# Attention, routed experts and a PReLU layer on one core: the high and low parts of an expert's tokens in one product, an expert's matrices in two halves of tiles

## The reference

```python
# q, k, v [4, 12, 448, 64]
scores = scale * q @ k.T - log(S)
x = (1 / (1 + exp(-scores))) @ v                    # as [1792, 768]
# eight experts, 224 tokens each, given out by logits x @ w_gate in falling order
h = maximum(x[mask] @ w1[e], 0.0)                   # w1 [8, 768, 1024]
out[mask] = h @ w2[e]                               # w2 [8, 1024, 768]
h = out @ w_in                                      # [768, 2048]
g = maximum(h, 0) + alpha * minimum(h, 0)
return g @ w_out                                    # [2048, 768]
```

## Time and profile before

| | |
|---|---|
| median of 3 runs | 1016.87 us (1015.24 to 1021.43) |
| the profiled execution | 1018.44 us, its span 1016.8 us |
| TensorE busy | 992.3 us of the span, 98% |
| DVE, ACT, POOL busy | 562.4, 397.0, 180.8 us |
| share of the chain that ended last | TensorE 93%, DVE 3%, ACT 2% |
| granted TensorE clock | 0.999 |

### The profile page before, as it was taken

The page is one execution under the profiler, slowest core; times in us unless marked ns, Lnnn a source line. Parts: engine busy times, 40 slices in busy tenths (PEclk is TensorE's granted clock), DMA queues, the critical chain, the costliest instruction groups (busy, mean ns, idle before and its releaser), DMA issues.

```text
span 1016.8 us, 16391 instructions
## 1 busy us (share of the span) xinstructions
PE 992.3 (98%) x6510; PEld 851.8 (84%) x6510; DVE 562.4 (55%) x1282; ACT 397.0 (39%) x642; POOL 180.8 (18%) x197
## 2 busy tenths in 40 slices
PE   7999999898999999999999999999999999999997
PEld 5555555467999999899999999999999999999996
DVE  4444343588678538948852873696358547221212
ACT  5767777511242223455222225531221455222212
POOL 0100000015420101244000024340101425000001
PEclk9999999999999999999999999999999999999999
DMA  9999985347598787676969646579785446976601
GB/s 212 273 277 270 253 259 175 139 154 255 143 322 320 230 190 250 230 185 204 368 235 242 238 146 174 176 267 341 229 241 181 142 129 197 372 244 216 217 1 55
DMA packets 122473, 222.48 MB, mean 219 GB/s; under 512 B 53056, under 2 KB 70752, under 8 KB 122064
## 3 DMA queue, kind: packets, MB, share of 16 engines
q1 hardware_dynamic: 89120, 121.14, 38.0%
q0 software_dynamic: 20304, 90.61, 28.1%
q10 hardware_dynamic: 12976, 9.70, 3.9%
HBM read 184.84 MB, written 36.58 MB: 218 GB/s over the span
## 4 chain that ended last, share of the span: by engine, by line
PE 93%; DVE 3%; ACT 2%; issue 1%; DMA 0%; POOLq 0%; POOL 0%; ACTq 0%; DVEq 0%
PE psum L1012 23%; PE psum L1026 22%; PE psum L959 11%; PE psum L989 10%; PE psum L740 7%; PE psum L724 7%; PE psum L708 2%; PE psum L954 2%; PE psum L984 2%; PE psum L841 1%; DVE hits L1606 1%; PE psum L906 1%; PE psum L766 1%; PE psum L894 1%; PE psum L758 1%
## 5 line engine op out<-in xcount | busy, mean ns | idle before, releaser
L1012 PE MATMUL psum<-y_high,unit 128*128 128x448 f32 x768 | 230.8, 369 | 0.5 <-DVE y_low L1520 0.4
L1026 PE MATMUL psum<-g_high,unit 128*128 128x448 f32 x756 | 228.0, 369 | 0.9 <-DVE g_low L1531 0.9
L1012 PEld LDWEIGHTS psum<-y_high,unit 128*128 128x128 f32 x768 | 144.3, 188 | 13.7 <-issue 1.2
L1026 PEld LDWEIGHTS psum<-g_high,unit 128*128 128x128 f32 x756 | 142.0, 188 | 14.2 <-DVE g_low L1531 1.9
L1012 PE MATMUL psum<-y_low,unit 128*128 128x448 f32 x384 | 140.7, 367 | 0.0
L1026 PE MATMUL psum<-g_low,unit 128*128 128x448 f32 x378 | 138.6, 367 | 0.0
L1210 ACT ACTIVATE above<-psum 128x448 f32<-128x448 f32 x64 | 34.9, 546 | 246.2 <-PE psum L1012 240.5
L1503 DVE TENSOR_TENSOR unit<-raw,unit 128x768 fp32r<-128x768 f32 (+1 forms) x106 | 109.6, 1059 | 38.7 <-ACT unit L1184 30.5
L1526 DVE SCALAR_TENSOR_TENSOR below<-below,neg_alpha,above 128x448 f32<-128x448 f32 x64 | 43.7, 683 | 148.9 <-ACT below L1211 148.7
L959 PE MATMUL psum<-x_high,unit 128*128 128x224 f32 x672 | 117.8, 276 | 1.0 <-issue 1.0
L989 PE MATMUL psum<-h_high,unit 128*128 128x224 f32 x672 | 115.7, 276 | 1.4 <-issue 1.4
(11 more groups left out here) (192 smaller groups left out, 1302.5 us busy)
## 6 DMA issues: line engine op xcount, KB each, us to landing
unit<-ffn_parts SPq DMA_DIRECT2D x120, 768.0 KB, 6.4
ffn_parts<-pre_parts POOLq DMA_DIRECT2D x24, 768.0 KB, 6.8
ffn_parts<-unit SPq DMA_DIRECT2D x8, 768.0 KB, 6.7
q_in<-in_q_dram SPq DMA_DIRECT2D x24, 224.0 KB, 4.7
v_in<-in_v_dram SPq DMA_DIRECT2D x24, 224.0 KB, 6.7
k_in<-in_k_dram SPq DMA_DIRECT2D x23, 224.0 KB, 6.2
pre_raw<-in_moe_w_in_dram ACTq DMA_DIRECT2D x12, 384.0 KB, 6.9
pre_raw<-in_moe_w_out_dram ACTq DMA_DIRECT2D x12, 384.0 KB, 6.3
```

What stands on the lines that cost most here:

```text
L1012: last = pe.matmul(psum[:, in_bank(m), 0:PAIR], w, y[:, c, :], start=(c == 0 and i == 0), stop=(c == DC - 1 and i == 2))
L1026: last = pe.matmul(psum[:, OUT_BANK + d, 0:PAIR], w, g[:, m % 2, :], start=(m == 0 and i == 0), stop=(m == (FC - 1 if q < GROUPS - 1 else ...
```

## The change

- `x_high` and `x_low` become one tile `x_both` with the two parts side by side, `h_high` and `h_low` become `h_both`. For each unit and tile, one product of 448 columns (weights high x both parts) and one of 224 (weights low x tokens high, into the second half of the same bank) take the place of three of 224. A tile of the result fills a bank and stands there as two halves of 224 columns, whose sum is the result.
- A bank now holds one tile, so `hidden` goes in two halves of 4 tiles and `returned` in two halves of 3, each over all units. The second half uses the banks of the first, and its first products wait until DVE has added the two sides of each (`h_added`, `y_added`). Units are given back in the second half only. Units of an expert are needed at twice the rate in a first half.
- DVE adds the two sides: `add_h`, 8 `tensor_reduce` for each expert, `add_y`, 6. Each reads 448 columns of PSUM, hopping between the sides, and writes 224 to SBUF. They stand first in DVE's steps. The relu, the rounding and the rests then read these sums in SBUF. y goes in 6 pieces of 224 columns, not 3 of 448.
- The rank passes have other steps; DVE's and ACT's splits of two steps reach less far ahead; the first row of fillers is 69, not 76; POOL gathers three units of w2 ahead of the second expert's tokens (in the groups after the first).
- Expert 0 and the PReLU layer keep their products.

```diff
-    BUSY_SEARCH, BUSY_FLAGS, BUSY_PLACES, BUSY_VALUES = 76, 11, 14, 10
+    BUSY_SEARCH, BUSY_FLAGS, BUSY_PLACES, BUSY_VALUES = 69, 11, 14, 10
...
-        x_high = [sb(f"x_high{i}", [128, DC, CAP], F32R) for i in range(2)]
-        x_low = [sb(f"x_low{i}", [128, DC, CAP], F32R) for i in range(2)]
+        x_both = [sb(f"x_both{i}", [128, DC, 2, CAP], F32R) for i in range(2)]
-        h_high = sb("h_high", [128, EC, CAP], F32R)
-        h_low = sb("h_low", [128, EC, CAP], F32R)
+        summed_h = ExitStack()
+        h_sums = sb("h_sums", [128, EC, 2, CAP], F32, summed_h)
+        summed_h.close()
+        h_both = sb("h_both", [128, EC, 2, CAP], F32R)
...
+        summed_y = ExitStack()
+        y_sums = sb("y_sums", [128, DC, PAIR], F32, summed_y)
+        summed_y.close()
...
         def prepared(s):
-            return {OWN - 2: OWN + 2, OWN - 1: OWN + 4}.get(s, 0) if s < OWN else s + LEAD + 1
+            if s < OWN:
+                return {OWN - 2: OWN + 2, OWN - 1: OWN + 4}.get(s, 0)
+            return s - s % STEPS + OWN + DC - 2 if s % STEPS in (OWN - 2, OWN - 1) else s + LEAD + 1
         SPLIT = [u for u in range(LAST) if is_own(u) and u >= OWN or is_late(u)]
...
                 if r == 2:
-                    passes, later = (21, 22, 23, 24, 28, 30, 31, 32), (34, 35, 37, 41)
+                    passes, later = (21, 24, 25, 28, 30, 31, 32, 33), (34, 35, 37, 41)
                 elif r == 3:
                     passes, later = (43, 45, 47, 48, 50, 51, 52, 53), (55, 57, 59, STEPS + 5)
                 elif r % 2 == 0:
-                    passes, later = (9, 11, 13, 16, 22, 24, 26, 28), (31, 32, 34, 38)
+                    passes, later = (22, 24, 26, 28, 30, 31, 33, 34), (36, 37, 39, 43)
                 else:
-                    passes, later = range(42, 50), (51, 52, 54, STEPS + 3)
+                    passes, later = (45, 46, 47, 48, 50, 51, 52, 53), (54, 55, 57, STEPS + 4)
                 PASS_AT[r] = [at + i for i in passes]
                 THR_AT[r], FLAGS_AT[r], IDX_AT[r] = [at + i for i in later[0:3]]
...
+            def three_terms(bank, w_high, w_low, both, first, final):
+                def high():
+                    return pe.matmul(psum[:, bank, 0:2 * CAP], w_high, both.rearrange("p a s -> p (a s)"),
+                                     start=first, stop=final, skip_group_check=True)
+                def low():
+                    return pe.matmul(psum[:, bank, CAP:2 * CAP], w_low, both[:, 0, :], start=False, stop=False,
+                                     skip_group_check=True)
+                if final:
+                    low()
+                    return high()
+                high()
+                return low()
+            def hidden(r):
+                M = EC // 2
+                for half in range(2):
+                    for c in range(DC):
+                        u = w1_unit(r, c)
+                        step = step_of(half, c, DC)
+                        if step is not None:
+                            rows_back(w1_unit(r, step))
+                            routing(w1_unit(r, step))
+                        if half == 0:
+                            if c == 0:
+                                if r == 1:
+                                    pe.wait_ge(first_split, DC // 2)
+                                else:
+                                    pe.wait_ge(sel_split, PIECES * (r - 1))
+                                if r % 2 == 0:
+                                    pe.wait_ge(in_taken, FC * (r // 2))
+                                    pe.wait_ge(out_taken, DC * (r // 2 - 1) + M - 1)
+                            pe.wait_ge(w_split, splits(u + 1))
+                        for i in range(M):
+                            m = M * half + i
+                            if half == 1 and c == 0:
+                                pe.wait_ge(h_added, h_sum(r, i))
+                            last = three_terms(H_BANK + i, *part(unit, u, m), x_both[r % 2][:, c], c == 0, c == DC - 1)
+                            if c == DC - 1 and m < EC - 1:
+                                last.then_inc(h_done, 1)
+                        if half == 1:
+                            last.then_inc(unit_used, 1)
+            def returned(r):
+                M = DC // 2
+                for half in range(2):
+                    for c in range(EC):
+                        u = w2_unit(r, c)
+                        step = step_of(half, c, EC)
+                        if step is not None:
+                            routing(w2_unit(r, step))
+                        if half == 0:
+                            if c == 0:
+                                if r == 1:
+                                    pe.wait_ge(y_split, y_ready(0, DC - 1))
+                                elif r % 2 == 1:
+                                    pe.wait_ge(y_added, y_sum(r - 1, DC - 1))
+                                else:
+                                    pe.wait_ge(rows_taken, ROWS * (r // 2))
+                            pe.wait_ge(h_split, EC // 2 * (r - 1) + c // 2 + 1)
+                            pe.wait_ge(w_split, splits(u + 1))
+                        for i in range(M):
+                            m = M * half + i
+                            if half == 1 and c == 0:
+                                pe.wait_ge(y_added, y_sum(r, i))
+                            last = three_terms(Y_BANK + i, *part(unit, u, m), h_both[:, c], c == 0, c == EC - 1)
+                            if c == EC - 1 and m < DC - 1:
+                                last.then_inc(y_done, 1)
+                        if half == 1:
+                            last.then_inc(unit_used, 1)
...
-                        pe.wait_ge(y_split, DC // 2 * (2 * q + 1) + c // 2 + 1)
+                        pe.wait_ge(y_split, y_ready(2 * q + 1, c))
...
+            def round_h(r, i):
+                act.wait_ge(h_added, h_sum(r, 2 * i + 1))
+                act.activation(h_both[:, 2 * i:2 * i + 2, HIGH, :], h_sums[:, 2 * i:2 * i + 2, LOW, :], ACT.Relu
+                               ).then_inc(h_rounded, 1)
...
+            def round_y(r, m):
+                own = slice(CAP * (r % 2), CAP * (r % 2) + CAP)
+                act.wait_ge(y_added, y_sum(r, m))
+                act.copy(y_high[:, m, own], y_sums[:, m, own]).then_inc(y_rounded, 1)
...
-                    if k == OWN * i + DC:
-                        round_h(2 * q + i)
-                    if k == OWN * i + OWN:
-                        round_y(2 * q + i)
+                    r = 2 * q + i
+                    if r > 0:
+                        for at, some in ((DC // 2, (0, 1)), (DC, (2, 3))):
+                            if k == OWN * i + at:
+                                for n in some:
+                                    round_h(r, n)
+                        for at, some in ((DC + EC // 2, (0, 1, 2)), (OWN, (3, 4, 5))):
+                            if k == OWN * i + at:
+                                for n in some:
+                                    round_y(r, n)
...
+            def both_sides(bank):
+                return psum[:, bank, 0:2 * CAP].rearrange("p (a s) -> p s a", a=2)
+            def add_h(r, m):
+                if m < EC - 1:
+                    dve.wait_ge(h_done, h_closed(r, m))
+                else:
+                    dve.wait_ge(unit_used, w1_unit(r, DC - 1) + 1)
+                dve.tensor_reduce(h_sums[:, m, LOW, :], both_sides(H_BANK + m % (EC // 2)), AX_X, ALU.add
+                                  ).then_inc(h_added, 1)
+            def split_h(r, i):
+                low = h_both[:, 2 * i:2 * i + 2, LOW, :]
+                dve.wait_ge(h_rounded, EC // 2 * r + i + 1)
+                dve.scalar_tensor_tensor(out=low, in0=h_sums[:, 2 * i:2 * i + 2, LOW, :], scalar=0.0,
+                                         in1=h_both[:, 2 * i:2 * i + 2, HIGH, :].bitcast(F32),
+                                         op0=ALU.max, op1=ALU.subtract).then_inc(h_split, 1)
...
+            def add_y(r, m):
+                own = slice(CAP * (r % 2), CAP * (r % 2) + CAP)
+                if m < DC - 1:
+                    dve.wait_ge(y_done, y_closed(r, m))
+                else:
+                    dve.wait_ge(unit_used, w2_unit(r, EC - 1) + 1)
+                dve.tensor_reduce(y_sums[:, m, own], both_sides(Y_BANK + m % (DC // 2)), AX_X, ALU.add
+                                  ).then_inc(y_added, 1)
+            def split_y(r, m):
+                own = slice(CAP * (r % 2), CAP * (r % 2) + CAP)
+                dve.wait_ge(y_rounded, y_ready(r, m))
+                dve.tensor_tensor(y_low[:, m, own], y_sums[:, m, own], y_high[:, m, own].bitcast(F32),
+                                  ALU.subtract).then_inc(y_split, 1)
...
+                        if r > 0:
+                            for at, some in ((DC // 2, (0, 1, 2, 3)), (DC, (4, 5, 6, 7))):
+                                if k == OWN * i + at:
```

(15 more changed lines are left out.)

145 lines of the change are left out of this document (61 added, 84 removed).

## The result

The changed kernel takes 1044.33 us (median of 4 runs, 1041.98 to 1047.47) where the kernel before takes 1017.68: ratio 1.026, 95% interval 1.0215 to 1.0306. The forecast was 1022 with a range of 1002 to 1036; it is slower, and by five times what the sum had. The profiled execution is the one of 1041.98, span 1040.3 against 1016.8: 23.5 us to account for, where the sum had 5.1.

A forecast was written before the change was run, and what follows sets the result against it. TensorE, busy 98% of the span, was taken as the bound. Experts' waits less products saved gave +6.4 us, fillers -1.3, net +5.1: 1018.44 to 1023.5 as profiled, 1022 in runs; range 1002 to 1036.

The forecast's parts named there:

- Products: Experts' matrices: a pair of 448 and 224 columns takes 0.308 us against 0.335 for three of 224, saving 18.1 us.
- The bound with 0.319: Cautious bound on the products' saving: a pair at 0.207 + 0.112 = 0.319 us saves 10.8 us.
- Fillers: First row of fillers, ahead of thr_rows: 7 fewer at 0.189 us each save 1.3 us.
- The boundaries and DVE's queue: Halves of h and y: TensorE waits for sums behind splits and passes; experts 1, 3, 5, 7 net +1.2, +0.5, +1.5, +0.2 us.
- The sum's length: DVE's adding of a tile's two sides: 0.62 us for each reduce of 448 columns.
- rival B: DVE's sums pay for hopping between sides, 0.93 us each: 1046 us in runs, chance 0.15.
- Experts 2, 4, 6: First experts: waits for tokens' rests and y's sums make each 37.1 us, +1.0 each, 3.0 in all.
- rival D: Weight units given back late, so the next come two us late in each expert: 1036 us, chance 0.08.
- What costs nothing: Moved passes and longer `later` steps in the PReLU layer, where DVE is often idle, and y's six rests: no cost.
- A wait that is added on TensorE is time lost, one for one: Throughout the kernel: TensorE, busy 98% of the span, loses exactly the length of each added wait.
- case A: DVE keeps up, only the least waits at the halves remain: -12.4 us, 1004.5 us in runs, chance 0.27.

The follow-up runs named there:

- the last mixed form: Kernel before with experts 1, 3, 5, 7 changed, second halves in other banks, DVE order and pass steps placed anew, 69 fillers: ratio 0.9871, then 0.9938 (1006.69 us).

## Why the prediction was wrong

- **Products.** Right in kind, mis-sized: 0.3135 a pair, not 0.308, so 14.5 us saved and not 18.1. The 224 takes 0.102 as read, but a 448 behind a 224 takes 0.211, not the 0.206 it takes among its own; no row of the kernel before had that order. The bound with 0.319 was on the safe side of it. The rule of the Trainium skill, "TensorE: Matmul & The Clock Gate", section "Wait — 56ns, not 53.3ns?", would have given an estimate of 1.7 us saved; 48 pairs in 15.04 us against 48 triples in 16.08 disagree.
- **Fillers.** Right: 1.8 us by themselves, 1.3 forecast.
- **The boundaries and DVE's queue.** Right in kind, and close in total, in part by luck: experts 1, 3, 5, 7 were to take 35.6, 34.3, 34.3, 32.6; without their half clock they take 35.7, 35.0, 34.6, 33.1. Of that the slower pair is 0.5 each. The waits themselves, from start to start and with the pace: at h 2.4, 1.4, 1.4, 1.5 against 3.0, 1.65, 1.65, 1.65; at y 2.3, 2.7, 2.3, 0.8 against 2.45, 2.45, 2.45, 1.3; and 0.7 in the middle of the second matrix, which the sum left out for expert 7. So the errors had both signs. The sum's length was right and rival B fell; no hop is paid on PSUM: 0.614 us. The Trainium skill, "Vector Engine (DVE) Microarchitecture Reference", on the access granule's adjacent pairs, has a case for either, both measured in SBUF; the trace, in PSUM, agrees with its case of one stream alternating between two regions.
- **Experts 2, 4, 6.** 37.1 forecast; 38.3 and, less the half clock, 38.2 for 4 and 6, 41.6 for 2. The slower pair is 0.5 of the difference. At h the pairs follow every 0.53 here too, 0.6 lost where 0.2 was left for it behind the six transposes; the waits for tokens are 1.6 against 1.4, y's 2.0 as forecast. Expert 2's late unit was rival D, which I priced evenly (2 us everywhere) and gave 0.08. It came once, where a 0.9 MB transfer stands ahead of a gather with little time left.
- **"What costs nothing", the moved passes: a step that failed in kind.** They cost the PReLU layer 2 to 3 us in each of two groups and 0.5 in a third, 5.0 in all; the kernel before with the new steps alone is 5 us slower, and the changed kernel with the old steps has PReLU layers 6.1 us shorter. DVE's busy share (55% of the span) said nothing on whether it is free where threshold, flags and rests of g are due.
- **The clock had no term at all: the other step that failed in kind.** "A wait that is added on TensorE is time lost, one for one" took every wait at its own length. The clock fell four times, 6.8 us, more than the whole forecast loss. The earlier trace rows had 1.00 in every window, with no wait of over 1.4 us in an expert; that was true of the few old waits, and I carried it over to eight waits of 1.1 to 3.3 us.
- **The range.** The faster case A held 0.27 and drew the low end, while four losses (pair, late unit, passes, clock) could fall together. Each slower rival was priced alone, at 1036 to 1046; the measured 1044 is none of them, but for the most part the forecast with these four on top. That 1044 is near B's 1046 is chance. What tells most is that the loss is not in the products: with other banks for the second halves and the queues put in another order, the same products gain 8.7 us in three experts without a wait. No run has the changed kernel with only its banks changed, so how much of that is the banks' and how much the queues' is not shown.

What stays open: why the clock falls behind some waits of 1.3 to 2.5 us and not behind others of 1.6 and 3.3 in the same execution, and what makes the tokens' waits in the first experts. The shorter reach of the splits and the earlier gathers of w2 were never run by themselves.

## What to carry to other kernels

Where a change makes TensorE wait for its neighbours at a boundary, look first for other banks, so that no product waits for a sum just begun; only then count what is saved. Trace every queue in its order: a unit late for its split holds the sums behind it, though its product is far off. Work that is moved to a stage where its engine is "often idle" has a price there too, if TensorE waits for anything that stands behind it. And price added waits of TensorE with a fall of the clock behind some of them: 1.7 us each here, three behind the eight waits of over 1 us in the experts of the profiled execution.

## What the runs showed of the hardware

The clock: the runs of the changed kernel and its variants, all with waits of 1.5 us or more on TensorE, had mean clocks of 0.979 to 0.997, those of the kernel before and the last mixed form mostly 0.997 to 1.0. In the traces every fall in an expert or a PReLU layer came during a wait of TensorE or at most 2.1 us behind one. The shortest such wait was 1.28 us (expert 6 of the changed kernel); the last mixed form has waits of 1.52, 1.52, 1.56 and 2.9 us with no fall behind any. In expert 0 of the changed kernel the fall stood behind two waits of 1.0 and 0.9. The stretches were 3.4, 6.8 or 10.2 us long and not in the same place in each execution.

The same products of 448 columns ran at two paces. The PReLU layer of group 3 of the kernel before, to be read beside the row of 113.08 above:

```profile
887.22:1002.60 115.38, 115.38 (x558) 104.83 (x559) 22.11 (x34) 25.32 (x49) 0.00 (x0) 1.00 0.47 158
```

Same instructions, same clock, no wait in either: 206.8 and 202.7 ns a product. The distances from start to start repeat, 207, 206, 207 in the one and 207, 202, 203, 202, 199 in the other, for the whole stage; in the PReLU layers of the other groups both paces occur, and one gives way to the other where transposes or a wait interrupt the products. It is not the change that decides: the kernel before with 69 fillers, and with the new pass steps, runs this stage at the faster pace as well (112.9 us from its first to its last product of 448, where the trace above has 115.2). So 2% of a stage can differ between two kernels that are alike in it; no run here shows what decides it.
